# The expert products' slot loop in half slots of four chunks and six row counts, with VectorE clearing the second product's banks

## What is computed

```python
x = attention(q, k, v)            # 4 batches, 8 heads, 576 positions, head size 64; local windows, plain or dilated
# x: 2304 tokens x 512
logits = x @ w_gate; e_idx = argmax(logits)            # one of 8 experts for each token
out[mask] = gate_w * eom * (relu(x[mask] @ w1[e]) @ w2[e])   # for each expert e: 512 -> 1024 -> 512
h = out @ w_in; g = max(h, 0) + log1p(exp(-abs(h))); y = g @ w_out   # 512 -> 2048 -> 512, all tokens
```

## Time and profile before

| | us |
|---|---|
| median of 3 runs | 832.69 |
| lowest, highest | 825.91, 837.83 |
| the profiled execution | 831.72 |
| its span | 829.9 |
| TensorE (PE) busy | 770.0 |
| PE weight load busy | 695.9 |
| VectorE (DVE), ScalarE (ACT), GpSimd (POOL) busy | 424.5, 410.0, 173.3 |

### The profile page before, as it was taken

How to read it: one execution, slowest core, us unless ns; L and a number is a source line. 1 busy time by engine, 2 the same in 40 slices (tenths; PEclk the granted TensorE clock), 3 DMA queues, 4 the chain that set the end, 5 groups by cost and what they waited for, 6 DMA issues and landing times.

```text
span 829.9 us, 13450 instructions
## 1 busy us (share of the span) xinstructions
PE 770.0 (93%) x4640; PEld 695.9 (84%) x4641; DVE 424.5 (51%) x854; ACT 410.0 (49%) x1041; POOL 173.3 (21%) x172
## 2 busy tenths in 40 slices
PE   5999995498989999999679999999999999999996
PEld 3667664498989999999669999999989999999995
DVE  8885986754534667665345343334343334334332
ACT  3885984244544566745345353344335335335332
POOL 6220220543360547634100010010001001001001
PEclk9999997599999999999879999999999999999999
DMA  9567502235443566755300010000000000000000
GB/s 261 160 187 270 203 0 114 77 131 174 142 166 132 196 220 200 230 176 199 130 2 1 0 39 0 0 25 13 0 0 38 0 0 38 0 0 38 0 0 38
DMA packets 27890, 74.70 MB, mean 90 GB/s; under 512 B 4737, under 2 KB 12945, under 8 KB 27345
## 3 DMA queue, kind: packets, MB, share of 16 engines
q1 hardware_dynamic: 20624, 53.52, 19.6%
q0 software_dynamic: 6224, 16.03, 5.9%
q10 hardware_dynamic: 1008, 4.73, 1.4%
HBM read 64.81 MB, written 9.46 MB: 89 GB/s over the span
## 4 chain that ended last, share of the span: by engine, by line
PE 89%; DVE 6%; issue 3%; ACT 1%; POOL 0%; ACTq 0%; DVEq 0%
PE bank L564 13%; PE bank L566 13%; PE bank L565 13%; PE bank L587 8%; PE bank L589 8%; PE bank L585 8%; PE bank L574 4%; PE bank L578 4%; PE bank L576 4%; PE bank L452 4%; PE bank L476 2%; PE bank L489 2%; PE bank L462 2%; PE bank L553 1%; PE bank L448 1%
## 5 line engine op out<-in xcount | busy, mean ns | idle before, releaser
L1099 DVE SCALAR_TENSOR_TENSOR g_sb<-bank,soft 128x384 f32<-128x384 f32 x96 | 53.5, 557 | 239.8 <-ACT soft L839 239.8
L835 ACT ACTIVATE soft<-bank 128x384 f32<-128x384 f32 x96 | 47.3, 492 | 213.9 <-PE bank L566 213.9
L564 PE MATMUL bank<-x_hi,w_hi 128*128 128x384 f32 (+2 forms) x448 | 145.6, 325 | 7.1 <-issue 6.0
L566 PE MATMUL bank<-x_hi,w_lo 128*128 128x384 f32 (+2 forms) x448 | 144.8, 323 | 0.0
L565 PE MATMUL bank<-x_lo,w_hi 128*128 128x384 f32 (+2 forms) x448 | 144.6, 323 | 0.0
L1053 DVE TENSOR_TENSOR w_lo<-raw,w_hi 128x1024 fp32r<-128x1024 f32 x72 | 98.0, 1365 | 31.3 <-ACT w_hi L761 30.3
L424 POOL DMA_INDIRECT out<-y_sb,out_rows_i x18 | 17.3, 963 | 413.8 <-ACT y_sb L846 410.2
L564 PEld LDWEIGHTS bank<-x_hi,w_hi 128*128 128x128 f32 x448 | 85.4, 191 | 10.7 <-issue 6.8
L565 PEld LDWEIGHTS bank<-x_lo,w_hi 128*128 128x128 f32 x448 | 85.4, 191 | 2.1
L566 PEld LDWEIGHTS bank<-x_hi,w_lo 128*128 128x128 f32 x448 | 85.2, 190 | 0.0
L790 ACT ACTIVATE h_hi<-bank 128x384 fp32r<-128x384 f32 x64 | 31.5, 492 | 101.1 <-PE bank L566 101.0
(11 more groups left out here) (165 smaller groups left out, 1569.1 us busy)
## 6 DMA issues: line engine op xcount, KB each, us to landing
raw<-we SPq DMA_DIRECT2D x64, 512.0 KB, 3.5
x_tokens<-x_sb ACTq DMA_DIRECT2D x6, 768.0 KB, 5.1
v_sb<-vw SPq DMA_DIRECT2D x4, 1024.0 KB, 11.8
raw_m<-wm POOLq DMA_DIRECT2D x8, 512.0 KB, 4.1
raw<-wm SPq DMA_DIRECT2D x8, 512.0 KB, 3.5
q_sb<-qT SPq DMA_DIRECT2D x4, 768.0 KB, 8.4
k_sb<-kT SPq DMA_DIRECT2D x8, 384.0 KB, 10.1
v_sb<-vw SPq DMA_DIRECT2D x4, 512.0 KB, 4.6
```

Source lines behind the costliest of these rows:

```text
L564: nc.tensor.matmul(bank_[:, 0:rows], hi[:, w], x_hi[:, k, 0:rows], start=(k == 0), stop=False)
L566: last = nc.tensor.matmul(bank_[:, 0:rows], lo[:, w], x_hi[:, k, 0:rows], start=False, stop=(k == KC - 1))
```

## The change

- The slot code on TensorE covers four chunks (half a slot) and runs twice in an inner loop over `half`. It exists for six row counts: 384, 352, 320, 288, 256, 224. Of the eight slots here, 280 and 278 tokens now run as 288 rows in place of 320, and 196 and 203 as 224 in place of 256.
- There is one loop over all 13 slots with a test `slot < used + E`; the fourth copy of the code is gone.
- Since the first chunk of both halves shares code, no p2 has a start flag. VectorE sets the four banks to zero after ScalarE copied them (zero_y), and p2 waits for that.
- The rows' parts lie in two buffers (x_parts, chosen by the slot's parity). Transposes are made in threes, one in each of four places of a slot. Rows are gathered in halves of 256 columns, and GpSimd multiplies them by the gate factors (scale_half).
- The gate factors no longer pass through memory: a second set of 18 matmuls with the one-hot matrix puts them in place (scale_ps), in three bf16 pieces. The three row gathers of factors per slot and the store are gone; the first slot's rows are scaled by VectorE (scale_first).
- Raw weights have their own ring of 4 places, separate from w_lo. A load waits for the split of the chunk four before it, and ScalarE's split waits for the p2 that used the place.
- The output order's 18 scatters move behind the slots on GpSimd.

```diff
-SIZES = (SLOT, 320, 256)
+SIZES = (SLOT, 352, 320, 288, 256, 224)
...
-RING = FC1
-AHEAD = 4
-HRING = 4
...
+RING = 4
+HALF = FC1 // RING
+AHEAD = RING - 1
+HRING = 3
...
-                    sp.wait_ge(g2_done, slot * FC1 + (f + 1))
-                    sp.dma_start(raw[:, f, :], we[expert, f]).then_inc(raw_loaded[f], 16)
+                    sp.wait_ge(w_lo_done, slot * FC1 + (f - RING + 1))
+                    sp.dma_start(raw[:, f % RING, :], we[expert, f]).then_inc(raw_loaded[f % RING], 16)
...
+            def scale_half(slot, h):
+                q = 2 * (slot - 1) + h
+                pool.wait_ge(halves_loaded[h], 16 * TPS * slot)
+                if q:
+
+                    pool.wait_ge(rows_t_done, FIRST_T + 2 * q)
                 for j in range(TPS):
                     c = slot * TPS + j
...
+                    nc.gpsimd.tensor_scalar(xs_sb[:, j, :], landing[:, j, h, :], row_scale[:, c:c + 1], None, ALU.mult
+                                            ).then_inc(rows_scaled, 1)
...
+            for s in range(1, E + 1):
+                for h in range(2):
+                    scale_half(s, h)
+                    if s < E:
+                        halves_scaled(s, h)
+                        load_half(s + 1, h)
+                    elif not h:
+                        split_mlp_chunk(s - 2)
...
+                    if not h:
+                        load_mlp_chunk(s - 1)
+                    elif 1 < s < E:
+                        split_mlp_chunk(s - 2)
+            split_mlp_chunk(E - 1)
...
+            def product2_columns(i, hi, lo, done, rows, zeroed=None):
+                h = i % 2
                 for k in range(KC):
+                    if zeroed is not None:
+                        pe.wait_ge(y_zeroed, zeroed + (k + 1))
...
+            def half_slot_products(slot, half, parity, rows):
+                first = slot * FC1 + half * RING
+
+                def p1(i):
+
+                    pe.wait_ge(w_lo_done, first + (i + 1))
+                    pe.wait_ge(h_lo_done, first + (i - 2 + 1 + H_CREDIT))
+                    product1(h_ps[i % 2], w_hi[:, i, :], w_lo[:, i, :], g1_done, rows, bass.ds(parity, 1),
+                             (x_lo_done, slot * KC) if i == 0 else None)
+
+                def p2(i):
+
+                    pe.wait_ge(h_lo_done, first + (i + 1 + H_CREDIT))
+                    product2_columns(i, w_hi[:, i, :], w_lo[:, i, :], g2_done, rows, slot * KC if i == 0 else None)
+
+                p1(0)
+                p1(1)
+                p2(0)
+                p1(2)
+
+                pe.wait_ge(x_lo_done, slot * KC + half * 2 + FIRST_X)
+                pe.wait_ge(rows_scaled, slot * (2 * TPS) + half * TPS + TPS)
+                transpose_rows(0)
+                p2(1)
+                p1(3)
+                transpose_rows(1)
+                p2(2)
+                p2(3)
...
+                def from_size(half, n):
                     if n == len(SIZES) - 1:
-                        slot_products(slot, SIZES[n])
+                        half_slot_products(slot, half, parity, SIZES[n])
                         return
                     with pe.If(taken > SIZES[n + 1]):
-                        slot_products(slot, SIZES[n])
+                        half_slot_products(slot, half, parity, SIZES[n])
                     with pe.If(taken <= SIZES[n + 1]):
-                        from_size(n + 1)
-
-                from_size(0)
-
-            with pe.Fori(0, E) as slot:
-                sized_slot(slot)
-            with pe.Fori(0, OVER) as n:
-                with pe.If(n < used):
-                    slot_products(n + E, SLOT)
+                        from_size(half, n + 1)
+
+                with pe.Fori(0, HALF) as half:
+                    from_size(half, 0)
...
+            with pe.Fori(0, SLOTS) as slot:
+                with pe.If(slot < used + E):
+                    slot_products(slot)
...
+                    nc.scalar.activation(h_hi[:, f % 2, :], h_ps[f % 2][:, 0:SLOT], ACT.Relu).then_inc(h_hi_done, 1)
...
+                    c = f + AHEAD
+                    act.wait_ge(g2_done, slot * FC1 + (c - RING + 1 + G2_CREDIT))
+                    split_hi(c % RING, raw_loaded[c % RING], slot * (16 * HALF) + 16 * (c // RING + 1), w_hi_done)
...
+            def slot_parts(slot):
+                other = bass.ds((slot + 1) % 2, 1)
+                for f in range(FC1):
+                    dve.wait_ge(h_hi_done, slot * FC1 + (f + 1))
+                    nc.vector.scalar_tensor_tensor(h_lo[:, f % 2, :], h_ps[f % 2][:, 0:SLOT], 0.0,
+                                                   h_hi[:, f % 2, :].bitcast(F32), ALU.max, ALU.subtract
+                                                   ).then_inc(h_lo_done, 1)
+                    if f % RING >= 2:
+                        k = f // RING * 2 + f % RING - 2
+                        row_lo(other, k, t_ps[k % 2], slot * KC + (FIRST_X + k + 1))
+                    c = f + AHEAD
+                    split_lo(c % RING, slot * FC1 + (c + 1))
+                for k in range(KC):
+                    dve.wait_ge(y_copied, slot * KC + (k + 1 + PLACE_CREDIT))
+                    zero_y(k)
...
+            dve.wait_ge(scales_summed, 1)
+            step(V.tensor_copy(row_scale[:, :], scale_ps[:, 0:BLOCKS]))
+            step(V.tensor_tensor(row_scale[:, :], row_scale[:, :], scale_ps[:, BLOCKS:2 * BLOCKS], ALU.add))
+            V.tensor_tensor(row_scale[:, :], row_scale[:, :], scale_ps[:, 2 * BLOCKS:3 * BLOCKS], ALU.add
+                            ).then_inc(row_scales_ready, 1)
+            dve.wait_ge(row_scales_ready, 1)
+            scale_first(0)
+            for k in range(KC):
+                zero_y(k)
...
+            scale_first(2)
+            split_lo(0, 1)
+            for k in range(KC):
+                row_lo(slice(0, 1), k, first_t_ps[k], k + 1)
+            split_lo(1, 2)
+            split_lo(2, 3)
```

More of the change, by code:

```diff
@@ L290, in _ @@
                     slot_weights(n + E)
-            for r in range(RING):
-                sp.wait_ge(g2_done, used * FC1 + (E * FC1 + r + 1))
-                sp.dma_start(raw[:, r, :], wm[KEPT + r]).then_inc(tail_loaded[r], 16)
+            for v in range(TAIL):
+                sp.wait_ge(w_lo_done, used * FC1 + (E * FC1 + v - RING + 1))
+                sp.dma_start(raw[:, v % RING, :], wm[KEPT + v]).then_inc(raw_loaded[v % RING], 16)
         @block.gpsimd
@@ L776, in _, with row_part @@
-            for j in range(TPS):
-                act.wait_ge(first_rows[j], 32)
-                scale_rows(0, j)
-            def rows_hi(first, ks, banks):
-                for k in ks:
-                    act.wait_ge(rows_t_done, first + (k + 1))
-                    nc.scalar.activation(x_hi[:, k, :], banks[k % len(banks)][:, 0:SLOT], ACT.Copy).then_inc(x_hi_done, 1)
-            def slot_parts(slot, ahead):
-                start = act.value_load(start_i[0:1, bass.ds(slot, 1)], min_val=0, max_val=N)
+            def row_part(parity, n, k):
+                return x_parts[:, parity, n:n + 1, k, :].rearrange("p a n r -> p (a n r)")
```

398 lines of the change are left out of this document (208 added, 190 removed).

## The result

| us | before | changed |
|---|---|---|
| median (4 runs each, side by side) | 831.75 | 854.54 |
| lowest, highest | 825.91, 837.83 | 850.38, 856.93 |
| the profiled execution | 831.72 | 856.93 |
| its span | 829.9 | 855.2 |

The ratio is 1.0268, interval 1.0183 to 1.0353: the change makes the kernel slower. The median lies above the 838 forecast and within the range of 820 to 856. The profiled execution is the slowest of the changed kernel's four, 2.4 us above their median.

The account below looks back on a forecast made before the run. It took the slots to be bound by TensorE's matmul time, sequencer costs between slots and the gap before the last layer. Terms summed to +5.9 on the profiled 831.7, giving 837.6; the median stands 1.0 higher, predicted 838, range 820 to 856.

Parts of the forecast that it names:

- my likeliest case: Whole kernel: changed median within 2% (16.7 us) of the kernel before; chance 0.72.
- rows: Slot products: four slots lose 32 rows each, at 0.000417 us a row; -10.2 us.
- transposes and the rest: Slots: four blocks of three transposes replace two of six, slowing the products behind them; +1.4 us.
- first product: Routing's end: longer VectorE chain, with 0.8 us waiting for gate matmuls, delays the first slot's start by +0.5 us.
- stall 3.4: First slot: TensorE is out of work before the first h_lo is ready, 3.4 us (0 to 5).
- sequencer 11.0: Slot and half boundaries: row-count comparisons outlast the queued products; +11.0 us (+5 to +15).
- dear jumps 5.6: Slot code: four jumps to code not at hand cost 11.9 us against 6.3 before; +5.6 (0 to +12).
- half clock: Slots: lower clock behind gaps of some 7 and 3.6 us from the first jumps; +2.5 us (0 to +4).
- gap before the last layer: Slots' end: without the spare loop's code the last layer starts sooner; -8.3 us, 0 if jumps are dear again.
- the last gap stays: Rival, before the last layer: the jump behind the loop is dear again; 846 us, chance 0.1.
- if gaps in the slots are put down to GpSimd or VectorE: Slots: a stated sign that the prediction is wrong; no size given.
- GpSimd's scaling: Slots: each 256-column scaling on GpSimd takes 0.3 to 0.7 us, priced at nothing in the sum.

Follow-up runs that it names:

- a_tree: The changed kernel with its six row counts found by halving the list instead of one after the other; 848.1 us, ratio 1.0212 to the kernel before.
- a_three: The changed kernel with only the three old row counts (384, 320, 256) in its half-slot code; 834.5 us, ratio 1.0037 to the kernel before.
- b_four: The kernel before with a single slot loop and four row counts (384, 320, 288, 224) found by halving, whole-slot code; 859.6 us, ratio 1.0173.
- b_pad4: The kernel before with TensorE's sequencer loading the slot's token count four more times at each slot; 857.0 us, ratio 1.0157.
- c_f16: a_three with the one-hot matmuls in 16-bit floats of 11 bits, one token piece and two factor pieces; 842.9 us, ratio 1.0048 to the kernel before.
- a_four: The changed kernel with four row counts (384, 320, 288, 224) found by halving; 847.9 us, ratio 1.0058 to the kernel before.
- c_f16_224: c_f16 with row count 224 in place of 256; 845.1 us, ratio 1.0055 to the kernel before.
- a_again: The changed kernel itself, unedited, measured again on another chip; 864.3 us, ratio 1.0312 to the kernel before.
- the b_ kernels: Experiments that edit the kernel before, not the changed kernel: the single loop (measured twice), b_pad4 and b_four; ratios 0.995, 0.9951, 1.0157 and 1.0173.
- b_oneloop: The kernel before with one tested loop over all 13 slots and no spare loop; 837.6 us, ratio 0.995; repeated on another chip, 836.9 us, 0.9951.

## Why the prediction came out as it did

Against the profiled execution the sum was +5.9; measured is +25.2. The time lay in the range, near its upper end, but my likeliest case (within 2%, 0.72) did not come: the slow side, which had 0.20, did.

| term | predicted | measured |
|---|---|---|
| rows, 224 of them at 0.111 | -10.2 | -8.4 |
| transposes and the rest | +1.4 | +1.3 |
| first product | +0.5 | +4.7 |
| gaps: stall 3.4, sequencer 11.0, dear jumps 5.6 | +20.0 | +23.2 |
| half clock | +2.5 | +11.3 |
| gap before the last layer | -8.3 | -7.8 |
| last layer | 0 | +0.8 |

- **A little too high: the rows' gain.** That 224 rows stay on the line was assumed; a product of 224 rows took 0.111 and not 0.107, 1.8 us over two slots.
- **Right: the mechanism and its place.** Sequencer costs of 0.4 for each count passed, against a cover of some 16 products, gave 1.0 in the middle of a 224-row slot (measured 1.65) and, in order from the second boundary on, 0.4, 0.5, 2.0, 2.4, 1.7, 1.2 (measured 0.8, 0.5, 2.2, 3.0, 2.3, 2.0). Without the boundary at 207 us and the middle at 228, where dear jumps cover them, 10.4 was forecast and 14.7 came, some 0.5 each. Part of it is my own discount: by the formula the middle of a 224-row slot gives 3.2 - 1.7 = 1.5, and I wrote 1.0, "a little less" for the last body, but the trace has all five pairs. The rest is cover: there the sequencer comes to L686 1.4 us before the last product is through, not 1.7. That it is the ladder is shown by the five pairs in the gap itself and by a_tree; a_three takes code out as well.
- **Right: the dear jumps, with luck in the sum.** Three gaps of 2.6, 3.9 and 5.3 us at 186, 208 and 228 us, 11.7 in all, where I had 11.9, and none later. I had counted four jumps, the first at 1.7 and the others at 3.4 each; three larger ones came. This term rested on "paid at its first two visits"; b_four shows where the rule ends. By the two-page window of the Trainium skill ("Runtime: NRT & Kernel Launch", Instruction fetch mechanics) the jumps back over the loop would have stayed dear in the changed kernel too; none after 228 us was.
- **Right: the end of the slots** in this profile, 5.5 us. The rival "the last gap stays" came in the second profile all the same (14.25), by another cause than the one I named.
- **Too high: the stall before the first p2**, 3.4 for 1.37. Two stalls on h_lo of 0.85 and 0.81 in the 224-row slots were not in the sum at all: the stall that I had thought possible there was on the cleared banks, and these came from VectorE's splits beside GpSimd's subtraction. By my own sign ("if gaps in the slots are put down to GpSimd or VectorE") this part, 1.7 us, counts against me.
- **Too low, at no cost: GpSimd's scaling**, 1.0 us where I had 0.3 to 0.7.
- **Wrong, and the largest part of the miss (8.8 of 19.3 us): the clock.** The step that failed is "The first jumps now fall together into a gap of some 7 us, and another of 3.6: +2.5 for the clock". I priced the clock only behind the dear jumps, and gave my own seven gaps of 1 to 2.5 us none. In the trace each of the changed kernel's gaps at 314.2, 344.1, 374.7 and 406.1 (2.2, 3.0, 2.3 and 2.0 us) is followed within 3 us by 3.4 us at granted clock 0.50, which costs some 1.7. b_pad4 shows that gaps do it without any other edit. How much they cost is less sure: the same gaps cost 14.1 in this profile, 9.5 and 7.4 in two others, and by those the term would have been +6.7 or +4.6. The rows before the change could have told me: its one stretch lay behind one of its two gaps.
- **Wrong: the first product**, 0.5 for 4.7. The step is "some 0.8 of waiting for the gates' 18 matmuls". It should have been priced from a group of the kernel before that I did not bring in:

```profile
L536 PE MATMUL bank<-block_token,place_onehot 128*128 128x42 f16 x18 | 1.7, 264 | 6.7 <-DVE block_token L996 6.7
```

  At that rate 84 columns cost 3.4 us and 126 cost 5.1, an estimate (measured 3.0 and 4.3). c_f16, with 42 and 84 columns and three steps fewer, brings 4.9 back.

**What stays open: the late semaphore.** On the first chip the first copy followed the last product by 0.5 us in all four profiles, as in the changed kernel's first. On the other two it was 5.5 to 15.2 behind in all four kernels with the scatters behind the slots (a_four, c_f16, c_f16_224, a_again), and in time in the b_ kernels, whose scatters lie spread over the slots; both runs of the single loop had h_hi late instead, in slots where factors are gathered. This points to single-word indirect transfers (128 rows of 4 bytes) that delay TensorE's semaphore on some chips. But the chip is the plainer pattern. By the trace's records of semaphores, no count of TensorE between 150 and 450 us came over 0.3 us late in the two kernels' first profiles and the four of the first chip, and in all eight profiles of the other two chips some did, among them b_pad4 and b_four (at least 1.0) and, in slots where no single words move, a_four (1.0) and c_f16 (0.9). ScalarE's slow steps in a_again, and like ones in a_four, are no semaphore either. The test, c_f16 or the changed kernel with the eighteen scatters spread as before, was not run, nor was the kernel before profiled on these chips, so the cause is open. If the late copy went and nothing came in its place, c_f16 would fall from 843 to some 828, an estimate (20.2 - 5.5 = 14.7 us). The one version that beat the kernel before on its own chip, by half a per cent, is b_oneloop.

## What to carry to other kernels

A finer choice of code pays only as long as the sequencer's work at a boundary stays below what its queued products cover: count pairs of comparisons x 0.4 us, and the fixed part, against the 12 to 16 products seen here, and remember that the shortest tiles have both the least cover and, in a ladder that begins at the large end, the most comparisons. Price every gap of two microseconds or more on TensorE for itself and for the low clock that may come behind it: 1.7 us a time where it came, a quarter to a half of all gaps in the three profiles of the changed slots. For a matmul whose columns lie apart, and for the write that would bring them together, look up both rates before moving the spacing from one to the other.

## What the runs showed of the hardware that was not expected

- Eighteen one-hot matmuls at the lower clock, columns 36 bytes apart: 1.68 us for 42, 3.0 for 84, 4.34 for 126 columns, about 1.9 to 2.2 ns a column; side by side 1.48 for 84, 1.0 ns a column. VectorE writing 1512 16-bit elements with spaced addresses: 6.65 us for 0.95.
- The same gaps (29.5, 29.5, 29.6 us) cost 14.1, 7.4 and 9.5 us of half clock in three profiles.
- A loop of six half-slot bodies of some 230 instructions, or three of 430, keeps its code: no 16 KB instruction transfer from 232 us to the end of the changed kernel's slots. With four of 430, branches went on taking 3.5 to 7.4 us up to the last slot, beside 23 such transfers.
- A semaphore count of TensorE reached ScalarE 14.7 us after the matmul that raised it on the third chip, and 9.9 us on the second; on the first, and in the two kernels' first profiles, none came over 0.3 us late.
- VectorE's subtraction of 128 x 1024 float32 took 1.23 us with GpSimd idle and about 2.9 beside GpSimd's subtraction of the same size.
